# Attention feeding a mixture of experts and an FFN: numerators through ScalarE's copy, the division on GpSimd, and a new place for early low parts and two weight pieces

## The reference

```python
def phi(x):
    proj = np.einsum('bhsd,df->bhsf', x, w_phi)
    proj = proj - np.max(np.abs(proj), axis=-1, keepdims=True)
    return np.concatenate([np.exp(proj), np.exp(-proj)], axis=-1)
q_p, k_p = (phi(q), phi(k))
kv = np.einsum('bhsf,bhsd->bhfd', k_p, v)
z = np.sum(k_p, axis=2)
num = np.einsum('bhsf,bhfd->bhsd', q_p, kv)
den = np.einsum('bhsf,bhf->bhs', q_p, z)[..., None] + 1e-06
return num / den
```

## Time and profile before

| | |
|---|---|
| three runs, median (lowest to highest) | 909.52 us (904.52 to 909.9) |
| the profiled execution | 900.01 us, its span 898.3 us, mean granted clock of PE 0.994 |
| busy in the span | PE 875.0 us (97%), DVE 430.7 (48%), ACT 294.0 (33%), POOL 123.0 (14%) |
| attention (0 to about 208 us), early step (to about 240 us), the rest | PE busy 59.96 of the first 64 us, 47.97 of the next 49 us, 28.56 of 29 us from 211 on |

### The profile page before, as it was taken

The page is one execution under the profiler, slowest core; times in us unless marked ns, Lnnn a source line. Parts: engine busy times, 40 slices in busy tenths (PEclk is TensorE's granted clock), DMA queues, the critical chain, the costliest instruction groups (busy, mean ns, idle before and its releaser), DMA issues.

```text
span 898.3 us, 16710 instructions
## 1 busy us (share of the span) xinstructions
PE 875.0 (97%) x6432; PEld 794.5 (88%) x6433; DVE 430.7 (48%) x875; ACT 294.0 (33%) x479; POOL 123.0 (14%) x145
## 2 busy tenths in 40 slices
PE   8999999999999999999899999999999999999996
PEld 6776859588999999999899999999999999999996
DVE  5688888997587434443456422222222222222222
ACT  4555545652356333222444321121121112112111
POOL 1010203033234221125200010010000001001001
PEclk9999999999999999999999999999999999999998
DMA  8614614021754444328633720030020002000000
GB/s 280 201 54 176 225 53 158 2 81 40 256 149 119 80 79 65 69 30 183 153 128 119 178 88 1 1 106 1 1 70 35 0 25 80 0 0 36 1 1 36
DMA packets 37185, 75.37 MB, mean 84 GB/s; under 512 B 8176, under 2 KB 24688, under 8 KB 35472
## 3 DMA queue, kind: packets, MB, share of 16 engines
q1 hardware_dynamic: 32832, 56.07, 23.5%
q0 software_dynamic: 3488, 17.85, 5.4%
q10 hardware_dynamic: 816, 0.79, 0.3%
HBM read 51.06 MB, written 23.64 MB: 83 GB/s over the span
## 4 chain that ended last, share of the span: by engine, by line
PE 85%; DVE 8%; issue 3%; ACT 2%; DMA 1%; POOL 0%; DVEq 0%; POOLq 0%; SPq 0%; ACTq 0%
PE ps L1025 11%; PE ps L1027 10%; PE ps L1026 10%; PE ps L1040 5%; PE ps L1041 5%; PE ps L1039 5%; PE ps L927 4%; PE ps L928 4%; PE ps L929 4%; PE ps L940 3%; PE ps L942 3%; PE ps L941 3%; PE ps L768 3%; PE ps L823 2%; PE ps L728 2%
## 5 line engine op out<-in xcount | busy, mean ns | idle before, releaser
L1025 PE MATMUL ps<-xnH,blkH 128*128 128x384 f32 x576 | 194.6, 338 | 3.3 <-DVE blkL L1692 2.3
L1027 PE MATMUL ps<-xnH,blkL 128*128 128x384 f32 x576 | 194.2, 337 | 0.0
L1026 PE MATMUL ps<-xnL,blkH 128*128 128x384 f32 x576 | 194.1, 337 | 0.0
L1699 DVE TENSOR_TENSOR sg<-sg,ps 128x384 f32<-128x384 f32 x72 | 39.9, 554 | 246.6 <-ACT sg L1258 246.6
L1258 ACT ACTIVATE sg<-ps 128x384 f32<-128x384 f32 x72 | 35.4, 491 | 253.2 <-PE ps L1027 253.2
L1025 PEld LDWEIGHTS ps<-xnH,blkH 128*128 128x128 f32 x576 | 108.8, 189 | 7.5 <-issue 4.7
L1026 PEld LDWEIGHTS ps<-xnL,blkH 128*128 128x128 f32 x576 | 108.9, 189 | 2.7
L1027 PEld LDWEIGHTS ps<-xnH,blkL 128*128 128x128 f32 x576 | 108.8, 189 | 0.0
L1040 PE MATMUL ps<-blkL,hH 128*128 128x512 f32 x216 | 84.9, 393 | 0.0
L1041 PE MATMUL ps<-blkH,hL 128*128 128x512 f32 x216 | 84.8, 393 | 0.0
L1039 PE MATMUL ps<-blkH,hH 128*128 128x512 f32 x216 | 84.6, 391 | 0.0
(11 more groups left out here) (219 smaller groups left out, 1552.5 us busy)
## 6 DMA issues: line engine op xcount, KB each, us to landing
stage<-in_ffn_w SPq DMA_DIRECT2D x12, 768.0 KB, 4.3
xin<-xs_dram SPq DMA_DIRECT2D x9, 578.2 KB, 9.9
xs_dram<-zrow SPq DMA_DIRECT2D x8, 578.2 KB, 8.0
qT<-in_q SPq DMA_DIRECT2D x4, 1152.0 KB, 6.5
xnH_dram<-xoH SPq DMA_DIRECT2D x8, 576.0 KB, 3.5
xnL_dram<-xoL SPq DMA_DIRECT2D x8, 576.0 KB, 4.9
xnH<-xnH_dram SPq DMA_DIRECT2D x6, 768.0 KB, 4.9
xnL<-xnL_dram SPq DMA_DIRECT2D x6, 768.0 KB, 6.3
```

The lines of the kernel that those rows point to most:

```text
L1025: e.matmul(o, hi, xnH[par][:, c, :], start=(c == 0), stop=False)
L1026: e.matmul(o, hi, xnL[par][:, c, :], start=False, stop=False)
L1027: last = e.matmul(o, lo, xnH[par][:, c, :], start=False, stop=(c == KC - 1))
```

## The change

1. The numerators of a full query tile are copied from PSUM to a new buffer `x5n` (two of them, for tiles of even and odd number) by ScalarE, behind the exponentials of its slot (`copy_numerators`). The packed tile's are copied by VectorE at the start of its `normalise`.
2. `normalise` computes denominators and routing products from `x5n`. The multiplication L1364 is gone from VectorE; GpSimd's `set_aside` does it in the place of its copy (`x5n` times `rd` into `x5s`). `rd` has two buffers. `copy_numerators` and `normalise` wait for GpSimd and for `lgp` of the tile two before.
3. PE waits for ScalarE's copy (`act_N`) in the place of `dve_N`, and for the packed tile for `dve_N`, now set by VectorE's copy.
4. In the tail, VectorE's `take_rows` goes ahead of slot (B, 1), that is ahead of the fourth and the packed tile's normalisation.
5. The low parts of weight pieces 6 and 7, until now in slot 9 of the last batch and slot (B, 0), go behind `early_low(2)` and `early_low(3)`. PE's early step starts with 6 low pieces and waits for all 8 before the outputs of chunk 4.

The core of the diff (names of tiles and semaphores left out):

```diff
-        split_slots_dve = [(B - 1, sl) for sl in (1, 2, 5, 6, 7, 8, 9)] + [(B, 0)]
+        split_slots_dve = [(B - 1, sl) for sl in (1, 2, 5, 6, 7, 8)]
...
             def set_aside(b, j):
-                n = rows_of(j)
-                e.wait_ge(s["dve_N"], b * NJ + (j + 1))
+                at = (b, NJ + j)
+                e.wait_ge(s["dve_rd"], nkq(at) * 2)
                 settle(e, "carry_pool")
-                if j < NJ - 1:
-                    e.tensor_copy(x5s[0:n, j, 0:DM], x5[0:n, j, :]).then_inc(s["pool_x"], 1)
+                if not packed(at):
+                    e.tensor_tensor(x5s[:, j, 0:DM].rearrange("p (h d) -> p h d", d=D), x5n[:, j % 2, :, 0:D],
+                                    rd[:, j % 2, :].unsqueeze(2).to_broadcast([P, H, D]), ALU.mult)\
+                        .then_inc(s["pool_x"], 1)
...
                     elif at[1] > NJ + 1:
-                        e.wait_ge(s["dve_N"], nkq((at[0], at[1] - 2)))
+                        e.wait_ge(s["act_N"], nfull((at[0], at[1] - 2)))
...
+                    if m == 6 and begin > 0:
+                        e.wait_ge(s["sp_lo"], PIECES)
...
-                once(0, 0)
+                e.wait_ge(s["sp_hi"], PIECES)
+                e.wait_ge(s["sp_lo"], PIECES - 2)
                 hidden(0, 0, 0)
                 hidden(0, 0, 1)
-                e.wait_ge(s["dve_N"], B * NJ)
+                e.wait_ge(s["dve_N"], B)
...
+            def copy_numerators(at):
+                j = at[1] % NJ
+                e.wait_ge(s["pe_N"], nkq(at))
+                if not (isinstance(at[0], int) and at[0] == 0 and j < 2):
+                    e.wait_ge(s["pool_x"], aside_of(two_before(at)))
+                    e.wait_ge(s["dve_lp"], nkq(two_before(at)))
+                e.activation(x5n[:, j % 2, :, :].rearrange("p (b h) e -> p b (h e)", b=2),
+                             num_of(at).rearrange("p b h e -> p b (h e)"), ACT.Copy)\
+                    .then_inc(s["act_N"], 1)
...
+                if is_q(g2) and not packed(g2):
+                    copy_numerators(g2)
                 if sl == 5 and not (isinstance(b, int) and b == 0):
...
+                if packed(at):
+                    e.wait_ge(s["pe_N"], nkq(at))
+                    e.wait_ge(s["dve_lp"], nkq(two_before(at)))
+                    e.tensor_copy(x5n[:, j % 2, 0:HALF, :], num_of(at)[:, 0, :, :]).then_inc(s["dve_N"], 1)
+                    e.wait_ge(s["dve_N"], at[0] + 1)
+                else:
+                    e.wait_ge(s["act_N"], nfull(at))
...
-                e.tensor_tensor(x5[:, j, 0:heads * D].rearrange("p (b h d) -> p b h d", b=banks, d=D),
-                                num[:, :, :, 0:D], r4.unsqueeze(3).to_broadcast([P, banks, 4, D]), ALU.mult)\
-                    .then_inc(s["dve_N"], 1)
...
-            slot(B, 1)
             with e.If(early > 0):
                 take_rows(0, XT_FIRST)
...
+            slot(B, 1)
             slot(B, 2)
             slot(B, 3)
             early_low(0)
             slot(B, 4)
             early_low(1)
             early_low(2)
+            split_low(PIECES - 2, 0, PIECES - 1)
             route_3(B)
...
             early_low(3)
+            split_low(PIECES - 1, 0, PIECES)
```

More of the change, by code:

```diff
@@ L96, in build_program @@
         kvs = att("kvs", [P, KC, 4, VA])
-        x5 = att("x5", [P, NJ, DM])
+        x5n = att("x5n", [P, 2, H, VA])
         x5s = att("x5s", [P, NJ, ROW])
@@ L231, in build_program @@
                 "act_kv dve_kv pe_C act_cv dve_cv",
-            "queries: transposed, features, numerators, 1 / denominators, rows; logits by head, logits":
-                "pe_pT act_Q pe_N dve_rd dve_N dve_lp dve_g dve_L",
+            "queries: transposed, features, numerators, on chip, 1 / denominators; logits by head, logits":
+                "pe_pT act_Q pe_N act_N dve_N dve_rd dve_lp dve_g dve_L",
             "routing: steps, experts, exponentials, ranks, ranks read, places": "r_chain r_hot r_exp pe_R r_evac r_pos",
-            "rows set aside, scattered, their buffers free": "pool_x scat c_vec",
+            "rows normalised, scattered, their buffers free": "pool_x scat c_vec",
             "the early step's flag, its steps; the table": "r_early e_chain tab_set",
@@ L309, in nkq, with nfull @@
             return at[0] * NJ + (at[1] % NJ + 1)
+        def nfull(at):
+            return at[0] * (NJ - 1) + (at[1] % NJ + 1)
         def num_of(at):
@@ L314, in num_of, with two_before, aside_of @@
             return ps[:, first:first + 2, 0:4 * VA].rearrange("p b (h e) -> p b h e", e=VA)
+        def two_before(at):
+            j = at[1] % NJ
+            return (at[0], at[1] - 2) if j > 1 else (at[0] - 1, NS - 1 - j)
+        def aside_of(at):
+            return at[0] * (NJ + 1) + (NJ + 1 + at[1] % NJ + 1 + packed(at))
         def settle(eng, name):
@@ L591, in set_aside @@
             def set_aside(b, j):
-                n = rows_of(j)
-                e.wait_ge(s["dve_N"], b * NJ + (j + 1))
+                at = (b, NJ + j)
+                e.wait_ge(s["dve_rd"], nkq(at) * 2)
                 settle(e, "carry_pool")
-                if j < NJ - 1:
-                    e.tensor_copy(x5s[0:n, j, 0:DM], x5[0:n, j, :]).then_inc(s["pool_x"], 1)
-                else:
-                    e.wait_ge(s["pool_x"], b * (NJ + 1) + (NJ + 1 + j))
-                    settle(e, "carry_pool")
[L600 to L604, removed]
+                if not packed(at):
+                    e.tensor_tensor(x5s[:, j, 0:DM].rearrange("p (h d) -> p h d", d=D), x5n[:, j % 2, :, 0:D],
+                                    rd[:, j % 2, :].unsqueeze(2).to_broadcast([P, H, D]), ALU.mult)\
+                        .then_inc(s["pool_x"], 1)
+                    return
+                e.wait_ge(s["pool_x"], b * (NJ + 1) + (NJ + 1 + j))
+                settle(e, "carry_pool")
+                for g in range(2):
+                    rows = rows_half(g)
+                    e.tensor_tensor(x5s[0:REM, j, g * HALF * D:(g + 1) * HALF * D].rearrange("p (h d) -> p h d", d=D),
+                                    x5n[rows, j % 2, 0:HALF, 0:D], rd[rows, j % 2, 0:HALF].unsqueeze(2)
+                                    .to_broadcast([REM, HALF, D]), ALU.mult).then_inc(s["pool_x"], 1)
+                    e.wait_ge(s["pool_x"], b * (NJ + 1) + (NJ + 1 + j + 1 + g))
+                    settle(e, "carry_pool")
             def scatter(b):
@@ L745, in key_sums @@
                     e.wait_ge(s["in_v"], at[0] * (16 * (NJ - 1)) + 16 * (NJ - 1 - FIRST_V))
-                    e.wait_ge(s["dve_N"], at[0] * NJ - 1)
+                    e.wait_ge(s["act_N"], at[0] * (NJ - 1))
                     settle(e, "carry_pe")
@@ L771, in key_sums @@
                 if j == 0 and not first:
-                    e.wait_ge(s["dve_N"], at[0] * NJ)
+                    e.wait_ge(s["dve_N"], at[0])
                     settle(e, "carry_pe")
@@ L1117, in slot @@
                         .then_inc(s["act_kv"], 1)
+                g2 = before_slot(b, sl, 2)
                 if is_k(g1):
@@ L1346, in normalise @@
             def normalise(at):
[L1347 to L1350, removed]
+                j, heads = at[1] % NJ, HALF if packed(at) else H
+                num, r = x5n[:, j % 2, 0:heads, :], rd[:, j % 2, 0:heads]
+                if not (isinstance(at[0], int) and at[0] == 0 and j < 2):
+                    e.wait_ge(s["pool_x"], aside_of(two_before(at)))
@@ L1354, in normalise @@
                 links = (nkq(at) - 1) * 2
-                r4 = rd[:, 0:heads].rearrange("p (b h) -> p b h", b=banks)
-                e.tensor_scalar(r4, num[:, :, :, VW], 1e-6, None, ALU.add).then_inc(s["dve_rd"], 1)
+                e.tensor_scalar(r, num[:, :, VW], 1e-6, None, ALU.add).then_inc(s["dve_rd"], 1)
                 e.wait_ge(s["dve_rd"], links + 1)
-                e.reciprocal(rd[:, 0:heads], rd[:, 0:heads]).then_inc(s["dve_rd"], 1)
+                e.reciprocal(r, r).then_inc(s["dve_rd"], 1)
@@ L1359, in normalise @@
                 e.wait_ge(s["dve_rd"], links + 2)
[L1360 to L1363, removed]
-                e.tensor_tensor(x5[:, j, 0:heads * D].rearrange("p (b h d) -> p b h d", b=banks, d=D),
-                                num[:, :, :, 0:D], r4.unsqueeze(3).to_broadcast([P, banks, 4, D]), ALU.mult)\
-                    .then_inc(s["dve_N"], 1)
+                e.tensor_tensor(lgp[:, 0:heads, :], num[:, :, D:VW], r.unsqueeze(2).to_broadcast([P, heads, 2 * E]),
+                                ALU.mult).then_inc(s["dve_lp"], 1)
```

4 lines of the change are left out of this document (2 added, 2 removed).

## The result

| | median | lowest to highest | runs |
|---|---|---|---|
| before | 906.43 us | 904.27 to 909.90 | 11 |
| after | 913.63 us | 909.61 to 916.48 | 11 |

The ratio is 1.0078, with a 95% interval of 1.0062 to 1.0095: 7.2 us slower. The forecast was 911.5 us, or +2.0 us as a difference. The change is slower, as forecast, but it costs three and a half times what I summed up. That 911.5 lies only 2.1 us from the measured 913.63 is luck: it stood on the median of three runs of before, 909.52, and with eleven that median is 906.43, 3.1 us lower. The profiled execution of after took 915.05 us (span 913.4, mean granted clock 0.992).

A forecast was written before the change was run, and what follows sets the result against it. PE, busy 97% of the span, was taken as the bound, leaving only its stops to win. Turns +1.65 and early step +0.35 gave +2.0 us on 900.01, or 911.5 from the median 909.52; range 903.0 to 917.0.

The forecast's parts named there:

- the inventory of 6.9 us: PE's stops at the turns and before the early step, with the clock: 6.9 us, all the change can reach.
- The hand-off: Attention turns: VectorE starts `normalise` only after ScalarE's 0.71 us copy; each turn costs 0.55 us more, three turns +1.65.
- The sign that I named: Sign of being right: VectorE's `normalise` starts 0.6 us behind PE's numerators, with ScalarE as releaser.
- The upper bound: GpSimd's multiplication of 512 numbers in attention: 1.4 us taken, 2.8 at most.
- The 0.1 for contention: VectorE's `lgp`, read from SBUF beside GpSimd's work, slowed by 0.1 us a normalisation, bounds 0 and 0.3.
- The rival in which GpSimd binds: GpSimd's multiplication takes 2.8 us and delays copies at the turns: 914.1 us, up to 920; chance 0.10.
- The early step: After attention: 3.05 us won before chunk 0, given back by waits before chunks 2 and 6, net 0.35 lost.
- The clock rival: The stop before chunk 6 makes the clock fall again, 1.59 us more: 913.1 us; chance 0.22.
- 1.59 more, 3.05 in all: Early step's start: 1.45 us won from the shorter stop plus 1.59 because the clock stays up, 3.05 together.
- The sum: Whole kernel: +1.65 for the turns and +0.35 for the early step, +2.0 us.
- The relief rival: The hand-off costs VectorE nothing, stops vanish, clock stays: 6.4 us faster, 903.1; chance 0.30 together with a half case.

The follow-up runs named there:

- e1: The kernel before, unchanged, profiled a second time: 904.49 us, ratio 0.9985 to the kernel before.
- e5: The kernel before plus the attention part, but VectorE reads PSUM directly and ScalarE copies for GpSimd a slot later; tail of before: 905.00 us, ratio 0.9987.
- e9: The attention part alone on the kernel before, with the division given back to VectorE and GpSimd only copying: 911.71 us, ratio 1.0103.
- e3: The kernel before with the tail part alone (items 4 and 5): 909.15 us, ratio 1.0034.
- e4: The kernel after, its tail kept, but VectorE reads PSUM directly and ScalarE copies for GpSimd a slot later: 907.36 us, ratio 1.0013.
- e2: The kernel after with items 4 and 5 undone, so the attention part alone: 907.89 us, ratio 1.0030.
- e11: The kernel of e5 timed anew in 12 runs: 902.55 us, ratio 0.9998 to the kernel before.
- e8: The kernel before, with the first two batches' scatters held until the next batch's first query tile's numerators are made: 908.44 us, ratio 1.0027.
- e6: The kernel before with `take_rows` ahead of slot (B, 1) alone, splits in their old places: 905.87 us, ratio 0.9994.

## Why the prediction was right or wrong

**What bounds the kernel.** Right in kind: PE is at 96% of the span and every part of the change acted through PE's stops. Wrong in one basis: the inventory of 6.9 us came from one execution of 900.01 us. Its 1.96 us stop and the 1.59 us of half clock behind it aren't there in e1, which has 0.99 us and the full clock. I saw that the profiled execution was 9.5 us under the median and still took its stops for the kernel's.

**`normalise`.** Right: 1.07 us against 1.03 predicted, and the packed copy 0.48 against 0.49 to 0.52.

**The inventory of stops** left one out: in the last turn 0.54 us ahead of 0.55 and 0.73, for ScalarE's `tile_high` (e1 has it too). It changes no term of the forecast.

**The hand-off.** Right in mechanism and in the copy (0.71 us), mis-sized in latency. I let ScalarE begin 0.05 us behind PE's end. In e1 the big group of numerators ends at 110.80 + 1.34 = 112.14 and `tile_low` starts at 115.30, 3.16 later. In after it ends at 113.01; timeline of ScalarE there:

```profile
113.32 0.71 ACT L1121 ACTIVATE x5n<-ps 128x648 f32<-128x648 f32 x1 [2.61 <-PE ps L839]
```

The copy starts 0.31 us behind, `normalise` 1.06 behind instead of 0.81, and `tile_low` at 116.53, 3.52 behind: 0.36 later than before where I had 0.18. The next `tile_low` follows after 5.35 us instead of 4.95, 0.40 more where I had 0.37. A turn costs 0.34 + 0.41 = 0.75 us, not 0.55. The turn after the first batch costs 0.99 (2.03 against 1.04) and the last 0.62 (0.84 + 1.59 against 0.54 + 0.55 + 0.72): +2.4 us for +1.65. The sign that I named, a start 0.6 us behind PE's numerators, didn't agree with my own sum, which has 0.81.

**GpSimd.** The upper bound fell: 1.06 us, under the 1.4 that I took. The 0.1 for contention was put on the wrong operation: `lgp` took 292 ns in e1 and in after, where it is nearly through when GpSimd starts. But contention there is. In after the packed tile's small copy `lgr` takes 0.40 us where e1 has 0.17, and `tile_low` is lengthened in e5 as shown, while the sum over heads, which reads one operand, takes 0.37 to 0.38 us in after with all of it beside GpSimd's multiplication, and 0.36 in e1. The Trainium skill's rule ("GPSIMD Engine Reference", section "Key points") names VectorE instructions with two inputs in SBUF, and `tile_low` in e5 agrees with it (0.80 and 1.18 us for 0.68). In after it cost almost nothing because of where the operations fall. The rival in which GpSimd binds is out, and e9 shows the reverse: its division is the part that pays.

**The early step.** The new stops came where they were put, sized 0.22, 1.40 and 1.69 us against 0.5, 1.1 and 2.3: 3.3 us where I had 3.9. The clock rival is out too, since the stop it needed came 0.6 us shorter; windows of the kernel after behind the stops at chunk 2 and chunk 6:

```profile
227.00:228.00 1.00, 0.67 (x5) 0.70 (x6) 0.97 (x4) 0.00 (x0) 1.00 (x3) 1.00 0.00 0
228.00:229.00 1.00, 1.00 (x10) 1.00 (x9) 0.93 (x6) 0.00 (x0) 0.36 (x1) 1.00 0.00 0
...
243.00:244.00 1.00, 1.00 (x9) 1.00 (x9) 0.96 (x4) 0.00 (x0) 0.00 (x0) 1.00 0.07 17
```

The step that failed is "1.59 more, 3.05 in all": the gain was booked against a stop and a fall of the clock that a typical execution doesn't have. Against e1's 0.99 the tail costs 3.31 - 0.99 = +2.3 us, not +0.35. e3 gives 0.34%, 3.1 us, with an interval of 1.2 to 5.1.

**The sum** by measured terms is 2.4 + 2.3 = +4.7 us. The two parts timed alone give 0.64%, 5.8 us, and the whole 7.2. For the one pair of profiles, after and e1 (spans 913.4 and 903.4 us), the starts of the same matmuls show where most of the other 5.3 us is. Three falls of the clock that e1 doesn't have take 4.0 us: after lags by 1.70 us before the one at 151 us and by 2.86 behind it, by 3.65 and 4.97 around 206 us, by 8.31 and 9.84 around 311 us. From chunk 0 to the second group of chunk 6 after loses 3.9 us, where the stops alone give 3.1.

Whether the change brings the falls, two profiles can't say: after has four (at 96, 151, 206 and 311 us), e1 one, the first profile of before two (211 and 450 us), the others none to three, the kernel's start and end left out. The mean granted clock of every timed run is on record, however. It accounts for most of the spread between runs (correlation with the time -0.93 in the 11 of after, -0.94 in the 35 of before timed beside e1 to e4). Its mean is 0.9936 in after and 0.9950 in those runs of before (taken at another time), which at 0.8 us for 0.001 of clock is about 1.1 us, with a 95% interval that holds zero. With (1 - clock) times the time taken off each run, after still lies 6.0 us over before (907.05 against 901.06), and e2 and e3 lie 3.2 and 3.3 us over it. Of the 6.0 us the stops give 4.7 and the chunks beyond their stops 0.8. So most of the cost is PE's stops and not the clock. How much of the last 1 to 2 us of the measured 7.2 is clock, and whether the change brings it, stays open.

**The relief rival** (903.1 us) is out for this form of the change: its condition was that the hand-off costs VectorE nothing. e5 and e11 make that condition true, and the time still doesn't go below that of before by an amount that can be told.

## What to carry to other kernels

When a division of labour puts a second engine between the producer and the engine that PE is waiting for, price the whole chain (release of the copy, copy, release of the reader; here 1.06 us where the direct read began after 0.25) against what the reader is spared (0.44). Let the extra engine feed only those who are off the path. Where the extra work goes to GpSimd, look which VectorE operations it will lie beside: `tile_low` grew from 0.68 to as much as 1.18 us. And before a stop is booked as a gain, look whether it is there in a second execution: a profile that lies under all timed runs shows an execution in which other stops are missing, and the gain is read from the wrong inventory.

## What I hadn't expected of the hardware

PE stops in the middle of 64 matmuls that wait for nothing the profile shows, two or three times 0.3 to 1.1 us, in three of the four batches, while GpSimd's indirect scatter of the 576 rows before is under way. In e1 the DMA share in these microseconds is 0.87 to 1.05 in the first of the three batches, but 0.59 to 0.72 in the second and 0.28 to 0.54 in the third, and the first profile of before has 0.88 to 1.09 there without a stop; so full DMA engines alone don't make them. The stops moved by 7 us with the scatter in e8, and were absent in one execution of before. What holds PE there (the fetch of its instructions or something else) no run here tells.

The granted clock fell to the lower level (0.50) for some 3.4 us after the stops at 94 us in e1, and didn't after stops of 1.40 and 1.69 us in after. In the 13 profiles, the kernel's first 12 us left out, all four single stops of 1.96 us or more had a fall behind them (1.96 and 1.98 in the first profile of before, 2.00 in e6, 2.45 in e3). Of the 46 of 1.2 to 1.9 us two had one (1.66 at 309 us in after, 1.76 at 304 us in e3), and the longest, 1.89 and 1.83 us in e9, had none. So the length of the last stop alone didn't decide.
